# Linear attention and two feed-forward stages on one core: the rank's matmuls in column strips, and where the rank and the mixing stand in the order

## The reference, cut to what matters

```python
# attention, per batch (4), head (8) and step t (768); head_dim 48
f = 1 / (1 + exp(-f_logit))
state = f[t, :, None] * state + outer(k[t], v[t])
y[t] = q[t] @ state
# x: (batch, 768 tokens, 384 channels); U (768, 32), V (32, 768)
h = x.transpose(0, 2, 1) @ U @ V
u = x + h.transpose(0, 2, 1)                        # the low-rank mixing over tokens
x2 = u + maximum(u @ w_ch1, 0) @ w_ch2              # 384 -> 1536 -> 384
h2 = maximum(x2 @ w_in, 0)                          # 384 -> 1024
gate = sigmoid(conv over 3 tokens of h2)
out = (h2 * gate) @ w_out                           # 1024 -> 384
```

## Time and profile before

| | us |
|---|---|
| median of 3 runs | 738.42 (738.24 to 738.48) |
| the profiled execution, its time | 738.63 |
| its span, from first to last instruction | 736.7 |
| TensorE busy | 704.6 (96% of the span) |
| VectorE busy | 441.7 (60%) |
| ScalarE busy | 246.4 (33%) |
| GpSimd busy | 289.7 (39%) |

### The profile page before, as it was taken

How to read it: one execution, slowest core, us unless ns; L and a number is a source line. 1 busy time by engine, 2 the same in 40 slices (tenths; PEclk the granted TensorE clock), 3 DMA queues, 4 the chain that set the end, 5 groups by cost and what they waited for, 6 DMA issues and landing times.

```text
span 736.7 us, 23832 instructions
## 1 busy us (share of the span) xinstructions
PE 704.6 (96%) x10748; PEld 664.4 (90%) x10748; DVE 441.7 (60%) x706; ACT 246.4 (33%) x504; POOL 289.7 (39%) x262
## 2 busy tenths in 40 slices
PE   3888989999999999999999999999999999999998
PEld 3787789989999899999999889999999889999997
DVE  6895474573898464464598655365489832121875
ACT  1034524342236322212245431213134542121453
POOL 4862597691453234062253225145055311030432
PEclk9999999999999999999999999999999999999999
DMA  8331353412001110100201200110000000000000
GB/s 202 100 91 40 109 148 91 127 57 66 24 3 54 45 55 23 46 24 24 67 2 46 53 34 25 41 49 24 23 2 2 34 33 1 1 1 0 1 33 32
DMA packets 24293, 33.75 MB, mean 46 GB/s; under 512 B 5152, under 2 KB 17184, under 8 KB 24192
## 3 DMA queue, kind: packets, MB, share of 16 engines
q1 hardware_dynamic: 23184, 30.46, 15.3%
q10 hardware_dynamic: 1008, 1.77, 1.0%
HBM read 27.50 MB, written 4.72 MB: 44 GB/s over the span
## 4 chain that ended last, share of the span: by engine, by line
PE 72%; DVE 18%; issue 4%; ACT 3%; POOL 1%; DMA 1%; ACTq 0%; DVEq 0%; POOLq 0%
PE acc L700 8%; PE hb L681 7%; PE att L566 7%; PE hb L682 7%; PE hb L683 6%; PE acc L701 6%; PE acc L705 6%; DVE conv L1074 5%; DVE q_t L1002 3%; PE att L612 3%; DVE conv L1071 3%; PE acc L739 2%; PE hb L649 2%; PE acc L740 2%; DVE conv L1058 2%
## 5 line engine op out<-in xcount | busy, mean ns | idle before, releaser
L1044 DVE SCALAR_TENSOR_TENSOR r_lo<-hb,r_hi 128x386 fp32r<-128x386 f32 (+1 forms) x96 | 53.5, 557 | 193.2 <-ACT r_hi L864 193.2
L864 ACT ACTIVATE r_hi<-hb 128x386 fp32r<-128x386 f32 (+1 forms) x96 | 47.2, 492 | 260.1 <-PE hb L683 260.1
L1160 POOL TENSOR_TENSOR r_lo<-conv,r_hi 128x384 fp32r<-128x384 f32 x64 | 61.7, 964 | 168.6 <-ACT r_hi L879 168.6
L700 PE MATMUL acc<-r_hi,w_ch_hi 128*128 128x386 f32 (+1 forms) x288 | 103.8, 360 | 0.0
L1123 POOL TENSOR_TENSOR k_t<-k_t,blocks 112x512 f32<-112x512 f32 x60 | 81.5, 1361 | 55.2 <-PE att L566 45.0
L681 PE MATMUL hb<-u_hi,w_ch_hi 128*128 128x386 f32 (+1 forms) x288 | 98.3, 341 | 0.2 <-DVE r_lo L1044 0.2
L682 PE MATMUL hb<-u_hi,w_ch_lo 128*128 128x386 f32 (+1 forms) x288 | 97.5, 339 | 0.0
L701 PE MATMUL acc<-r_hi,w_ch_lo 128*128 128x386 f32 (+1 forms) x288 | 97.3, 338 | 0.0
L683 PE MATMUL hb<-u_lo,w_ch_hi 128*128 128x386 f32 (+1 forms) x288 | 96.9, 337 | 0.0
L566 PEld LDWEIGHTS att<-q_t,k_t 48*64 48x64 f32 (+3 forms) x3840 | 59.3, 134 | 25.6 <-issue 23.9
L1074 DVE SCALAR_TENSOR_TENSOR conv<-hb,convw,conv 128x384 f32<-128x384 f32 x128 | 79.1, 618 | 4.5
(11 more groups left out here) (134 smaller groups left out, 1343.4 us busy)
## 6 DMA issues: line engine op xcount, KB each, us to landing
v_p<-in_vn_dram SPq DMA_DIRECT2D x12, 384.0 KB, 3.6
out_dram<-ostage SPq DMA_DIRECT2D x24, 192.0 KB, 2.0
q_t<-in_qT_dram SPq DMA_DIRECT2D x21, 192.0 KB, 3.6
k_t<-in_kT_dram SPq DMA_DIRECT2D x21, 192.0 KB, 3.5
gates<-in_fT_dram SPq DMA_DIRECT2D x21, 192.0 KB, 3.5
ostage<-in_w_ch_dram SPq DMA_DIRECT2D x14, 192.0 KB, 2.8
conv<-in_w_ch_dram SPq DMA_DIRECT2D x10, 192.0 KB, 2.9
ostage<-in_w_out_dram SPq DMA_DIRECT2D x5, 192.0 KB, 2.5
```

The source lines that it names most:

```text
L700: pe.matmul(o, wh[:, j, ws], r_hi[:, s, 0:width], start=(j == 0), stop=False)
```

## The change

The rank's weights `mixu` hold U once, 32 columns. Unit t goes to strip t mod 3, that is, to PSUM partitions 32 (t mod 3) onwards, so that each strip sums two units. VectorE adds the three strips into a new tile `rank_sum` in SBUF (a copy and two additions). ScalarE casts `rank_sum` three times into the three parts of `rstack`, first, third, second; after the second of these casts VectorE subtracts in the third part. TensorE's first mixing waits for all three casts too. Two DMAs for the copies of `mixu` go.

In the order, the rank of the next batch stands behind the last `first2` and ahead of `second2` of chunk 12; it stood behind that. All three mixings stand between `second2` 14 and 15; two stood behind 13 and one behind 14. ScalarE's last sigmoid becomes a task of its own, `last_gate`, ahead of the casts of the rank (`rank_split`).

```diff
-            order += [("rank", 0, DUOS - 1)] + [("piece", FIRST + i) for i in range(3)]
+            order += [("rank", 0, DUOS - 1), ("rank_split", 0)] + [("piece", FIRST + i) for i in range(3)]
@@ in the loop over steps s
+            if b + 1 < B and s == 2 * N1 + 2 * N2 - 1:
+                order += [("rank", b + 1, j) for j in range(DUOS)]
             if q >= 0:
                 order.append(("second2", b, q))
@@
-        order += [("rank", b + 1, j) for j in range(DUOS)] * more + [("last2", b), ("second2", b, 2 * N2 - 3)]
-        order += [("mix", b + 1, i) for i in range(2)] * more + [("second2", b, 2 * N2 - 2)]
-        order += [("mix", b + 1, 2)] * more + [("second2", b, 2 * N2 - 1), ("out", b, 1)]
+        order += [("last_gate", b)] + [("rank_split", b + 1)] * more + [("last2", b)]
+        order += [("second2", b, 2 * N2 - 3), ("second2", b, 2 * N2 - 2)]
+        order += [("mix", b + 1, i) for i in range(CT)] * more + [("second2", b, 2 * N2 - 1), ("out", b, 1)]
@@ TensorE, rank_task
-                    pe.matmul(ring_bank(use, DM)[0:3 * RANK, :], mixu[:, t, :], x[:, t, :],
-                              start=(t == 0), stop=(t == UNITS - 1)).then_inc(rank_done, 1)
+                    g = slice(RANK * (t % 3), RANK * (t % 3) + RANK)
+                    pe.matmul(ring_bank(use, DM)[g, :], mixu[:, t, :], x[:, t, :], start=(t < 3), stop=(t >= 3),
+                              skip_group_check=True).then_inc(rank_done, 1)
@@ TensorE, mix_task
                     pe.wait_ge(rank_ready, b + 1)
+                    pe.wait_ge(rank_hi_ready, 3 * (b + 1))
@@ ScalarE
-                act.wait_ge(rank_done, UNITS * (b + 1))
+            def rank_split(b):
+                act.wait_ge(rank_summed, 3 * (b + 1))
                 if b > 0:
                     act.wait_ge(mix_done, 2 * CT * b)
-                nc.scalar.copy(rstack[:], ring_bank(ring_use(b, "rank", 0), DM)[0:3 * RANK, :]).then_inc(rank_hi_ready, 1)
+                for i in (0, 2, 1):
+                    nc.scalar.copy(rstack[RANK * i:RANK * (i + 1), :], rank_sum[:]).then_inc(rank_hi_ready, 1)
@@ VectorE
+                dve.wait_ge(rank_done, UNITS * (b + 1))
...
+                sums = [ring_bank(ring_use(b, "rank", 0), DM)[RANK * i:RANK * (i + 1), :] for i in range(3)]
+                nc.vector.tensor_copy(rank_sum[:], sums[0]).then_inc(rank_summed, 1)
+                for i in (1, 2):
+                    dve.wait_ge(rank_summed, 3 * b + i)
+                    nc.vector.tensor_tensor(rank_sum[:], sums[i], rank_sum[:], ALU.add).then_inc(rank_summed, 1)
+
+            def rank_split(b):
+                dve.wait_ge(rank_hi_ready, 3 * b + 2)
                 lo = slice(2 * RANK, 3 * RANK)
-                nc.vector.tensor_tensor(rstack[lo, :], ring_bank(ring_use(b, "rank", 0), DM)[lo, :], rstack[lo, :],
-                                        ALU.subtract).then_inc(rank_ready, 1)
+                nc.vector.tensor_tensor(rstack[lo, :], rank_sum[:], rstack[lo, :], ALU.subtract).then_inc(rank_ready, 1)
```

More of the change, by code:

```diff
@@ L301, in bass_gla_lowrank_mix_ffn_gated_conv_ffn @@
         wsplit = {"ch1": weight("ch1", [P, CT, FF1]), "ch2": weight("ch2", [P, N1, DM])}
-        mixu = sb("mixu", [P, UNITS, 3 * RANK])
+        mixu = sb("mixu", [P, UNITS, RANK])
+        rank_sum = sb("rank_sum", [RANK, DM])
         vstack = sb("vstack", [3 * RANK, S], F32R)
@@ L370, in bass_gla_lowrank_mix_ffn_gated_conv_ffn @@
         x_copied, x_copied_last = sem("x_copied"), sem("x_copied_last")
-        rank_done, rank_hi_ready, rank_ready = sem("rank_done"), sem("rank_hi_ready"), sem("rank_ready")
+        rank_done, rank_summed = sem("rank_done"), sem("rank_summed")
+        rank_hi_ready, rank_ready = sem("rank_hi_ready"), sem("rank_ready")
         mix_done, u_hi_ready, u_lo_ready = sem("mix_done"), sem("u_hi_ready"), sem("u_lo_ready")
@@ L457, in consts_mix @@
             def consts_mix():
+                sp.dma_start(mixu[:], mix_u.rearrange("(t p) r -> p t r", p=P)).then_inc(loaded_mix, 16)
                 for i in range(3):
-                    sp.dma_start(mixu[:, :, RANK * i:RANK * (i + 1)],
-                                 mix_u.rearrange("(t p) r -> p t r", p=P)).then_inc(loaded_mix, 16)
                     sp.dma_start(x[RANK * i:RANK * (i + 1), 2:4, :].rearrange("r a b -> r (a b)"), mix_v).then_inc(
@@ L645, in rank_task @@
                 if j == 0:
-                    pe.wait_ge(loaded_mix, 96)
+                    pe.wait_ge(loaded_mix, 64)
                     ring_free(use)
                 for t in range(2 * j, 2 * j + 2):
-                    pe.matmul(ring_bank(use, DM)[0:3 * RANK, :], mixu[:, t, :], x[:, t, :],
-                              start=(t == 0), stop=(t == UNITS - 1)).then_inc(rank_done, 1)
+                    g = slice(RANK * (t % 3), RANK * (t % 3) + RANK)
+                    pe.matmul(ring_bank(use, DM)[g, :], mixu[:, t, :], x[:, t, :], start=(t < 3), stop=(t >= 3),
+                              skip_group_check=True).then_inc(rank_done, 1)
             def mix_task(b, i):
@@ L814, in attention @@
                     if n == 0:
-                        act.wait_ge(loaded_mix, 96)
+                        act.wait_ge(loaded_mix, 64)
                         nc.scalar.copy(vstack[:], x[0:3 * RANK, 2:4, :].rearrange("r a b -> r (a b)")).then_inc(vstack_hi, 1)
@@ L913, in _ @@
                     piece(task[1])
-                elif kind == "rank":
-                    rank_task(*task[1:])
+                elif kind == "rank_split":
+                    rank_split(*task[1:])
                 elif kind == "mix":
@@ L923, in _ @@
                     first2(*task[1:])
+                elif kind == "last_gate":
+                    sigmoid2(task[1], 2 * N2 - 1)
                 elif kind == "last2":
-                    sigmoid2(task[1], 2 * N2 - 1)
                     cast2(task[1], 2 * N2 - 1)
@@ L1029, in rank_task @@
                     return
-                dve.wait_ge(rank_hi_ready, b + 1)
+                dve.wait_ge(rank_done, UNITS * (b + 1))
+                if b > 0:
+                    dve.wait_ge(rank_ready, b)
+                    dve.wait_ge(rank_hi_ready, 3 * b)
+                sums = [ring_bank(ring_use(b, "rank", 0), DM)[RANK * i:RANK * (i + 1), :] for i in range(3)]
[5 more added lines that the diff above has]
+                dve.wait_ge(rank_hi_ready, 3 * b + 2)
                 lo = slice(2 * RANK, 3 * RANK)
-                nc.vector.tensor_tensor(rstack[lo, :], ring_bank(ring_use(b, "rank", 0), DM)[lo, :], rstack[lo, :],
-                                        ALU.subtract).then_inc(rank_ready, 1)
+                nc.vector.tensor_tensor(rstack[lo, :], rank_sum[:], rstack[lo, :], ALU.subtract).then_inc(rank_ready, 1)
             def mix_task(b, i):
```

3 lines of the change are left out of this document (removed).

## The result

| | before | after |
|---|---|---|
| median of the executions run side by side, us | 740.73 (736.91 to 743.37, 20) | 736.98 (734.83 to 740.74, 20) |
| ratio, with its 95% interval | | 0.9951 (0.9935 to 0.9968) |
| profiled execution, us, and its span | 738.63, 736.7 | 736.76, 734.8 |

The change makes the kernel 0.49% faster, 3.6 us of 738.4. The forecast was 5.2 us. Beside the changed kernel the kernel before had a median of 740.73, not the 738.42 of its first three runs, so 733.2 and 736.98 must not be subtracted: the ratio is the measure.

A forecast was written before the change was run, and what follows sets the result against it. The length of TensorE's queue was taken to bound the kernel. Three boundaries at -6.5 us and the first batch at +1.3 gave -5.2 from the median 738.42: 733.2 us, range 731.6 to 737.2.

The forecast's parts named there:

- The rank at a boundary: At the ends of batches 0, 1 and 2, TensorE's rank falls from 3.87 to 1.70 us, gaining 6.5 in all.
- the 0.41: At each rank in strips, TensorE's change between whole array and parts costs 0.41 us, read from attention.
- Strips only in pairs: Rival for the rank's matmuls: only neighbouring strips overlap, 2.26 us plus 0.41 per boundary, 736.3 us in all; chance 0.10.
- No overlap: Rival for the rank's matmuls: strips don't overlap at all, so the kernel is slower, 742.3 us; chance 0.08.
- late chain: Rival at the boundaries: VectorE's operations or waits exceed the 0.8 us to spare; 736.2 with 1.8 us more; chance 0.07.
- The first batch: At the start no product covers the longer chain through ScalarE's casts: +1.3 us, between +0.6 and +2.
- the clock rises later: Rival in the first batch: strips or TensorE's longer wait delay full speed, costing 2.5 to 4.5 us, 736.7; chance 0.25.

The follow-up runs named there:

- neighbours: Changed kernel with units dealt to the strips as 0,1 / 2,3 / 4,5 instead of 0,3 / 1,4 / 2,5; ratio 0.9986 to the kernel before.
- casts_first: Changed kernel with ScalarE's three weight casts ahead of the sum's casts in the first batch; ratio 0.9957 to the kernel before.
- first_only: Strips in the first batch only, wide rank and TensorE's old order at the boundaries; ratio 1.0046 to the kernel before.
- after_again: The changed kernel measured once more, unaltered; ratio 0.9953 to the kernel before.
- busy_wait: Changed kernel with four wide matmuls, results unread, ahead of the first batch's first mixing; ratio 0.9942 to the kernel before.
- first_wide: Changed kernel with the first batch's rank wide as before, strips in batches 1 to 3; ratio 0.9904 to the kernel before, 732.71 us; repeated, 0.9904, 731.65 us.
- order_only: Changed kernel's new order, but the rank wide in all batches; ratio 0.9993 to the kernel before.
- wide_slow2: Changed kernel with the first batch's rank wide and ScalarE casting it five times before reporting; ratio 0.9955 to the kernel before.

## Why the forecast was wrong in size

**The rank at a boundary: right.** Forecast 1.29 + 0.41 = 1.70 us, a gain of 2.17 each, 6.5 in all. Measured: boundaries of 12.19 and 9.945, a gain of 2.25 each, 6.7 in all, so the strips with their change of mode cost 3.87 - 2.25 = 1.62 us, 1.29 and 0.33. The records start in groups of three every 0.32 us. One reading behind the 0.41 was wrong: the attention step at 272.94 moves 32 columns (`48x32` in the earlier trace rows), not 64. At the rank's rate its sixteen rounds are 0.43 us and not 0.86, and the change of mode would come out at 0.84. That step took 1.14 us, no less than the 1.16 of the one with 64 columns, so its time doesn't go by columns, and the 0.41 came close partly by luck. The Trainium skill's figure ("TensorE: Matmul & The Clock Gate", Part 3, measured speedup) of 2.38 gave 1.63 us as an estimate, and the trace agrees (1.62).

**Strips only in pairs: wrong**, by neighbours most clearly: even two matmuls of the same strip in a row leave the others free. The rule of the Trainium skill that had made this a rival ("PSUM — Partial Sum Buffer", Engine vs sequencer instructions: matmuls start in program order) doesn't describe the starts of these records; the one order and the other give 1.49 and 1.50 us.

**No overlap, late chain: didn't occur.** VectorE's three operations took 1.71 us (forecast 1.7). ScalarE's three casts took 1.58, 0.53 each and not the 0.46 of the two in the earlier trace rows. The subtraction ended at 598.76; the rank stood 0.38 later here, so that is 598.4 on the scale of the forecast's 598.5. The first mixing's matmul followed 0.7 us behind it (forecast 0.8).

**The first batch: the step that failed.** The term was +1.3, between +0.6 and +2. By profiles alone the strips there cost 178.2 (mean of the six kernels with strips and the gap, casts_first left out for its slow rank) less 175.0 = 3.2 us; the ratio of first_only says 3.4, and wide against changed 3.6 and 4.7. Of these 3.2 us, 1.8 lie ahead of the first product and 1.5 behind it (means 12.41 less 10.65, and 165.82 less 164.36). With 3.2 the sum is -6.7 + 3.2 = -3.5, and the changed kernel's three measurements gave -3.6, -3.5 and -2.4. Between the two profiles that this document shows it is even 178.23 - 173.85 = 4.4 us (-6.7 + 4.4, and the rank's start 0.35 later, give the -1.9 by which the spans differ). These 4.4 us are three parts.

- The first mixing's matmul: forecast 9.1 us behind the rank's start (82.1 - 73.01), 8.49 in the kernel before, 9.75 in the changed one. That is +1.3 against the forecast's +0.6. The last strips waited 0.33 for a copy of x and ended 6.2 us behind the rank's start instead of 5.8, and the attention half at 74.79 ran 1.64 us, not 1.15.
- From the first mixing's matmul to the first product: 2.84 us instead of 1.72, +1.1. The lower clock is 0.3 of it. The rest is ScalarE's order, as the forecast had it: the first `u_hi` cast comes 1.29 us behind the mixing instead of 0.50, VectorE's `u_lo` behind it, and the product's weights are loaded 0.12 to 0.16 us behind the end of the first `u_lo` in every profile but casts_first. In after_again, neighbours and busy_wait, whose first mixings ran at full clock, TensorE was done ahead of `u_lo` and it is 2.50 to 2.51 us. The first u_hi cast stands 11.0 us behind the rank (forecast 10.3), later by what the matmul was late.
- Behind the first product: 165.64 us to the boundary instead of 163.64, +2.0. The forecast's sum had nothing for this. The clock record is at 1.2 GHz until 89.56, 3.6 us behind the first product. In the table 163.60 to 163.66 are the three profiles whose clock was full from there on. Two of the kernels with a wide first rank aren't free of this either (first_wide and order_only, 165.1).

That it is 4.4 us here and 3.2 on average is because **the profile of before that I worked from was a fortunate one**: its 173.85 us is 1.2 under the mean of its kind. The three executions that gave 738.42 were fortunate too, 2.3 under the median of all twenty.

The rival "the clock rises later" had said that TensorE's longer wait "may have the same effect", at 2.5 to 4.5 us on top of the 1.3, and 736.7 in the end. That mechanism came, with less than its price: 3.2 to 3.5 in all, not 4.8. (That 736.98 was measured beside its 736.7 says nothing for it, since the kernel before stood at 740.73 then.) So the step that failed is the first batch's term. Its path, through ScalarE's casts, held, but it had the matmul's delay at 0.6 where 1.3 came, and the lower clock behind the wait, 2.3 us between the two profiles, at nothing. The mistake was to put the clock beside the forecast as a case of 0.25. The wait was in the forecast itself (mixing at 82.1 behind transposes at 79), and the trace already showed attention at half its speed in this part of the program.

**Still open.** What part of the 3.2 us is the wait and what part the clock in a typical execution: busy_wait took the fall behind the gap away but had a late clock ahead of it, the late u_hi cast and another fall behind it, and wide_slow2's only profile kept the clock full while the means of the others can't tell. Nor is it shown why first_wide and order_only lose 1.5 us behind their first product. Both have a fall of the clock there, for 3.4 us from 103 to 104 us on, as have after_again, neighbours and busy_wait at 105 to 106; the kernel before, with the same wait for attention's scores ahead of it, has none in its profile.

The row for first_wide, granted clock again third from the right:

```profile
104.00:108.00 4.00, 4.00 (x25) 3.94 (x18) 2.81 (x3) 0.00 (x0) 3.67 (x4) 0.58 0.66 204
```

## What to carry to other kernels

Splitting a narrow product into column strips pays where TensorE's queue is full and other work covers the chain that adds the strips up; decide it for each place, and leave the wide form where nothing covers (here: 0.9904 with the first batch wide, 0.9951 with strips everywhere). A gap of 3 us on TensorE early in a program is to be priced at its length and, as a case of its own, at what runs at the lower clock behind it: seven profiles with it had the fall, and one (wide_slow2) had not. Look as well for what stands in another engine's queue between the longer chain and the next use, here the weights' casts ahead of u_hi. Where a bracket names one releaser of several, look up in the kernel what the wait is for. And when a forecast starts from one profile, the start of a program is the part of it that varies: rest the sum on stretches that repeat, and take a range for the rest.

## What the runs showed of the hardware

- Three strips of 32 columns ran at full rate side by side, their passes 0.32 us apart in each strip, in both orders of issue that were tried (1.49 and 1.50 us for twelve records). The group cost 1.62 us of TensorE, 0.33 more than its four passes.
- An attention step of 64 records in quadrants took 1.14 us with 32 moving columns and 1.16 with 64.
- The granted clock in the first 110 us differs from execution to execution of one kernel, with stretches at 1.2 GHz of 3.4 to 20.5 us. At the end of the open gap of 2.9 us the strips' kernels had one in all seven profiles, and in all 84 executions the mean clock was under 0.998. In the one profile with the gap filled by matmuls it stayed full there, and behind a wide rank with a gap of 2.74 us too. In the table 3.1 to 3.6 us at the lower clock behind the first product cost 1.5 to 2.0 us (163.6 without, 165.1 to 165.6 with), and 5.4 us in two stretches 2.8 to 2.9 (after_again, neighbours).
- The final writes of the output landed in 2.0 us in one profile and in 3.7 and 3.5 in those of neighbours and casts_first, with the same code there.
